# Rewriting the opening of an attention, dense and routed feed-forward kernel: all four units loaded at once, eight PSUM banks, and weight splitting moved behind it

## The reference, cut to what matters

```python
# attention: B=4, H=8, S=768, D=48, a linear recurrence with decay w per head and channel
for t in range(S):
    kt, vt, rt = (k[:, :, t], v[:, :, t], r[:, :, t])
    cur = np.einsum('bhd,bhe->bhde', u[None] * kt, vt)
    y[:, :, t] = np.einsum('bhd,bhde->bhe', rt, state + cur)
    state = w[None, :, :, None] * state + np.einsum('bhd,bhe->bhde', kt, vt)
# dense part: 3072 tokens, 384 -> 2048 -> 384
h = np.maximum(x @ w_in, 0.0);  x = h * h @ w_out
# routed part: 8 experts, 384 tokens each by capacity, 384 -> 1024 -> 384
h = np.maximum(x[mask] @ w1[e], 0.0);  out[mask] = h @ w2[e]
```

## Time and profile before

| | us |
|---|---|
| median of 3 runs | 879.27 (878.26 to 884.58) |
| the profiled execution | 880.52 |
| its span | 878.7 |
| PE busy | 841.0 (96%) |
| DVE busy | 514.7 (59%) |
| ACT busy | 261.2 (30%) |
| POOL busy | 229.2 (26%) |
| mean granted clock of TensorE | 0.978 of full |

### The profile page before, as it was taken

How to read it: one execution, slowest core, us unless ns; L and a number is a source line. 1 busy time by engine, 2 the same in 40 slices (tenths; PEclk the granted TensorE clock), 3 DMA queues, 4 the chain that set the end, 5 groups by cost and what they waited for, 6 DMA issues and landing times.

```text
span 878.7 us, 15962 instructions
## 1 busy us (share of the span) xinstructions
PE 841.0 (96%) x6289; PEld 730.1 (83%) x6289; DVE 514.7 (59%) x1143; ACT 261.2 (30%) x479; POOL 229.2 (26%) x197
## 2 busy tenths in 40 slices
PE   7789999999999999999999999987999999999895
PEld 7678888888888888888888888877988989889795
DVE  7657645666566557666666444546667667666220
ACT  1223323333333333333433344310121222222221
POOL 5545332322243314222323400001031131131211
PEclk9779999999999999999999999988999999999998
DMA  6553212665655565555654455524664674674940
GB/s 209 180 168 89 72 58 87 196 200 190 202 191 194 194 217 185 201 196 195 200 198 150 146 187 186 188 78 150 232 228 155 225 259 153 226 252 138 361 142 28
DMA packets 64300, 156.08 MB, mean 178 GB/s; under 512 B 8289, under 2 KB 13793, under 8 KB 63841
## 3 DMA queue, kind: packets, MB, share of 16 engines
q1 hardware_dynamic: 57696, 140.90, 47.2%
q0 software_dynamic: 3072, 9.44, 3.3%
q10 hardware_dynamic: 3456, 4.72, 1.5%
HBM read 103.65 MB, written 51.38 MB: 176 GB/s over the span
## 4 chain that ended last, share of the span: by engine, by line
PE 87%; DMA 5%; DVE 3%; issue 2%; SPq 1%; ACT 1%; POOL 1%; POOLq 0%; ACTq 0%; DVEq 0%
PE ACC L1251 23%; PE U L1238 23%; PE U L1379 10%; PE ACC L1392 9%; PE P L1201 5%; PE P L1185 3%; PE P L1311 3%; DMA stage<-in_ew 3%; PE P L1198 2%; PE P L1226 1%; PE P L1209 1%; DMA stage<-in_w_in 1%; PE P L1215 1%; DMA rk<-x_rows,rowidx 1%; PE P L1136 1%
## 5 line engine op out<-in xcount | busy, mean ns | idle before, releaser
L859 DVE TENSOR_TENSOR hr<-hr 128x512 f32<-128x512 f32 x96 | 69.6, 725 | 123.6 <-ACT hr L675 123.0
L675 ACT ACTIVATE hr<-U 128x512 f32<-128x512 f32 x96 | 57.3, 597 | 240.9 <-PE U L1238 240.9
L1251 PE MATMUL ACC<-HH,WH 128*128 128x512 f32 x282 | 117.3, 416 | 0.0
L1238 PE MATMUL U<-XH,WH 128*128 128x512 f32 x288 | 114.7, 398 | 1.2 <-DVE XL L838 1.2
L1238 PE MATMUL U<-XL,WH 128*128 128x512 f32 x288 | 114.3, 397 | 0.0
L1238 PE MATMUL U<-XH,WL 128*128 128x512 f32 x288 | 114.1, 396 | 0.0
L1251 PE MATMUL ACC<-HH,WL 128*128 128x512 f32 x282 | 111.5, 395 | 0.0
L1251 PE MATMUL ACC<-HL,WH 128*128 128x512 f32 x282 | 111.0, 394 | 0.0
L583 POOL TENSOR_TENSOR tok<-tok,sdiag 128x384 f32<-128x384 f32 x24 | 30.5, 1272 | 246.2 <-DVE sdiag L865 246.2
L874 DVE TENSOR_TENSOR HL<-hr,HH 128x512 fp32r<-128x512 f32 x96 | 75.8, 789 | 21.8 <-ACT HH L659 21.6
L628 POOL DMA_INDIRECT rk<-x_rows,rowidx x24 | 24.9, 1039 | 230.5 <-DVE rowidx L1030 225.6
(11 more groups left out here) (178 smaller groups left out, 1580.3 us busy)
## 6 DMA issues: line engine op xcount, KB each, us to landing
stage<-in_ew SPq DMA_DIRECT2D x80, 256.0 KB, 3.0
split_high<-stage SPq DMA_DIRECT2D x80, 256.0 KB, 2.0
split_low<-stage SPq DMA_DIRECT2D x80, 256.0 KB, 2.1
WH<-split_high SPq DMA_DIRECT2D x40, 512.0 KB, 5.8
WL<-split_low SPq DMA_DIRECT2D x40, 512.0 KB, 6.7
tok<-in_tok SPq DMA_DIRECT2D x24, 576.0 KB, 5.8
rk<-in_rk SPq DMA_DIRECT2D x24, 448.0 KB, 5.0
stage<-in_ew SPq DMA_DIRECT2D x8, 512.0 KB, 10.3
```

What stands on the lines that cost most here:

```text
L675: nc.scalar.activation(hr[:, s % 2, :], U[s % 2][:, :], ACT.Relu).then_inc(relu_done, 1)
L859: tt(hr[:, s % 2, :], hr[:, s % 2, :], hr[:, s % 2, :], ALU.mult).then_inc(sq_done, 1)
L1238: ins = mm(U[s % 2][:, :], w_up((WH, WL)[a], k, s), (XH, XL)[b][:, q, k, :], start=(n == 0), stop=(n == 3 * KT - 1))
L1251: ins = mm(ACC[j][:, :], w_down((WH, WL)[a], s, j), (HH, HL)[b][:, s % HRING, :], start=(s == 0 and a == b), stop=(s == NF1 - 1 and a == 1))
```

## The change

The opening becomes code of its own, and `blocks` starts at body(1).

- **Loads.** Right after w, SP issues unit 0, u, the two masks and units 1 to 3. Units 2 and 3 have buffers borrowed for it (`hr`, the second stage buffer), and one weight chunk follows. Constants that only later stages use come last.
- **Tables.** The reciprocal over 112 x 512 goes; the second table is the first one read backwards, times a number per row. The copy goes too, since the scan writes the table directly. `Wt` is copied out of PSUM by ACT.
- **Banks.** Scores of even units go to P[0:2], of odd ones to U; Y has P[2], the state ACC[0], transposes ACC[1], warm-ups ACC[2]. AT has a second buffer.
- **State.** In the opening the state is zero: the product with S, `Sd` and the addition of the state go. ACT copies the update into S.
- **Weights.** The host lays them out by tile (`dw`); eight chunks of 1536 columns, up and down in turn. Chunk 0 is split in the opening, chunks 1 to 7 in block 1 at steps 0, 1, 3, 5, 6, 8 and 10. PE waits for chunk n ahead of its first use, at step 2n. In block 1, `load_unit(4)` and `(5)` are issued in the opening.

```diff
-WARM_UP = (104, 40, 24)
+WARM_UP = (72, 6, 16)
         def chunk_at(s, att, moe, post):
-            if att and not moe and s % 4 == 1:
-                return s // 4
-            if att and moe and not post and s % 4 == 0 and BATCH + s // 4 < W1CHUNKS:
-                return BATCH + s // 4
+            if moe and not post:
+                return {0: 1, 1: 2, 3: 3, 5: 4, 6: 5, 8: 6, 10: 7}.get(s)
             return None
@@ SP
-            load_unit(0, 0, 0)
-            load_unit(1, 1, 1)
-            load_weights(0)
-            load_weights(1)
-            load_weights(2)
-            for b in range(2, BATCH):
-                sp.wait_ge(y_mm, b - 1)
-                load_unit(b, b % 2, b)
-                load_weights(b + 1)
+            load_unit(1, 1, 1)
+            for b in range(2, BATCH):
+                sp.dma_start(opening_rk(b)[0:KP]..., rk_in[b, :, :]).then_inc(ld_late[b % 2], 16)
+                sp.dma_start(tok[:, b, :, :]..., tok_in[b, :, :]).then_inc(ld_tok[b], 16)
+            load_weights(0)
...
+            sp.wait_ge(y_mm, BATCH)
+            load_weights(1)
+            load_weights(2)
+            load_weights(3)
+            load_weights(4)
+            next_unit(1, 2)
+            load_weights(5)
+            next_unit(1, 3)
+            load_weights(6)
+            load_weights(7)
@@ DVE, tables
-            nc.vector.tensor_copy(pw[:, 0, :, :], pwx[:, :, 0:CHUNK]).then_inc(tab, 1)
-            nc.vector.reciprocal(pw[:, 1, :, :], pwx[:, :, 1:CHUNK + 1]).then_inc(tab, 1)
+            tt(wend[:, :], ends, wT[:, :], ALU.mult).then_inc(tab, 1)
+            nc.vector.reciprocal(winv[:, :], wend[:, :]).then_inc(tab, 1)
+            tt(w128[:, :], w64[:, :], wend[:, :], ALU.mult).then_inc(tab, 1)
+            tt(winv[:, :], winv[:, :], w64[:, :], ALU.mult).then_inc(tab, 1)
+            tt(pw[:, 1, :, :], pw[:, 0, :, ::-1], winv[:, :].unsqueeze(2).broadcast_to([KP, PAIRS, CHUNK]),
                ALU.mult).then_inc(tab, 1)
@@ DVE, opening (order of its queue)
+            opening_scale(0)
+            tt(etab, ...)
+            opening_scale(1)
+            opening_mask(0)
+            diagonal(0, 0)
+            opening_mask(1)
...
@@ PE, opening
+            for b in range(BATCH):
+                opening_y(b)
+                opening_state(b)
+                warm_up(WARM_UP[1], ACC[2])
+                if b + 2 < BATCH:
+                    opening_at_scores(b + 2)
+                if b == 0:
+                    pe.wait_ge(wt_done, 2)
+                opening_transpose(b)
+            warm_up(WARM_UP[2], ACC[2])
```

More of the change, by code:

```diff
@@ L216, in bass_attention_moe_routed_moe @@
         ld_const = sem("ld_const")
+        ld_urow = sem("ld_urow")
+        ld_masks = sem("ld_masks")
+        ld_late = [sem(f"ld_late{i}") for i in range(2)]
+        wt_done = sem("wt_done")
+        ones_set = sem("ones_set")
         ld_stage = [sem(f"ld_stage{i}") for i in range(2)]
@@ L320, in tasks_of @@
         def tasks_of(att, moe, post):
[L322 to L330, removed]
             if not att:
@@ L574, in unit @@
                 nc.gpsimd.tensor_tensor(r_t, r_t, urow[:, :], ALU.mult).then_inc(rku_done, 1)
+                if not state:
+                    pool.wait_ge(wt_done, 2)
                 after(pool, st_mm, u)
@@ L791, in _ @@
[L791 to L797, removed]
+            tt(wend[:, :], ends, wT[:, :], ALU.mult).then_inc(tab, 1)
+            dve.wait_ge(tab, 13)
@@ L839, in task, with diagonal @@
                        XH[cols].bitcast(f32), ALU.subtract).then_inc(xlo_done, 1)
+            def diagonal(c, b):
+                u = BATCH * c + b
+                dve.wait_ge(rku_done, u + 1)
+                after(dve, sv_done, u)
+                nc.vector.tensor_reduce(sdiag[:, :], tok[:, b, 0, :].rearrange(
+                    "p (h d) -> p h d", d=HDIM), AX.X, ALU.add).then_inc(sdiag_done, 1)
             def scale(c, b):
@@ L860, in body @@
                     if diagonal_at(s, att, moe) is not None:
[L861 to L866, removed]
+                        diagonal(c, diagonal_at(s, att, moe))
                     for n, kind, b in tasks_at(s, att, moe, post):
@@ L1136, in warm_up @@
                     mm(bank[:, 0:128], onesb[:, :], onesb[:, :], start=True, stop=True)
[L1138 to L1147, removed]
+            pe.wait_ge(ones_set, 1)
+            warm_up(WARM_UP[0], ACC[2])
             def evacuated(c, kind, b):
@@ L1163, in evacuated, with scores @@
                     pe.wait_ge(lg_done, u - 2 * BATCH + 1)
+            def scores(u, r_t, k_t, banks):
+                pe.wait_ge(scaled, u + 1)
+                for p in range(PAIRS):
+                    for par in range(2):
+                        lo = HP * par
+                        ins = mm(banks[par][:, p * 128:(p + 1) * 128], k_t[lo:lo + HDIM, p, :],
+                                 r_t[lo:lo + HDIM, p, :], start=True, stop=True)
+                        if p == PAIRS - 1:
+                            ins.then_inc(at_mm, 1)
@@ new lines, in state_update, with transpose_y @@
+            def state_update(u, bank, v_t):
+                pe.wait_ge(kw_done, u + 1)
+                for h in range(HEADS):
+                    lo, cols = HP * (h % 2), slice(h * HDIM, (h + 1) * HDIM)
+                    ins = mm(bank[lo:lo + HDIM, cols], KW[:, h, 0:HDIM], v_t[:, cols],
+                             start=True, stop=True)
+                ins.then_inc(st_mm, 1)
+            def transpose_y(u, bank):
+                pe.wait_ge(yadd_done, u + 1)
+                for k in range(KT):
+                    ins = nc.tensor.transpose(bank[:, k * 128:(k + 1) * 128],
+                                              ysum[:, k * 128:(k + 1) * 128], ident[:, :])
+                ins.then_inc(tr_mm, 1)
@@ new lines, in opening_at_scores, with opening_y @@
+            def opening_at_scores(b):
+                if b >= 2:
+                    pe.wait_ge(at_done, 2 * (b - 2) + 2)
+                scores(b, opening_rk(b)[:, 0], opening_rk(b)[:, 1], opening_scores(b))
+            def opening_y(b):
+                pe.wait_ge(at_done, 2 * b + 2)
+                pe.wait_ge(ld_tok[b], 16)
+                after(pe, yadd_done, b)
+                for h in range(HEADS):
+                    cols = slice(h * HDIM, (h + 1) * HDIM)
+                    ins = mm(P[2][:, cols], opening_at(b)[:, h, :], tok[:, b, 2, cols], start=True, stop=True)
+                ins.then_inc(y_mm, 1)
@@ new lines, in opening_state, with opening_transpose @@
+            def opening_state(b):
+                after(pe, st_done, b)
+                state_update(b, ACC[0], tok[:, b, 2, :])
+            def opening_transpose(b):
+                after(pe, xlo_done, b)
+                transpose_y(b, ACC[1])
+            opening_at_scores(0)
+            pe.wait_ge(tab, TAB_STEPS)
+            pe.wait_ge(ld_masks, 16 * 2)
+            for p in range(PAIRS):
+                ins = nc.tensor.transpose(ACC[1][:, p * KP:(p + 1) * KP], etab[:, p, :], ident[0:KP, 0:KP])
@@ L1178, in task @@
                 if kind == "AT1":
[L1180 to L1185, removed]
-                                     r_t[lo:lo + HDIM, p, :], start=True, stop=True)
-                            if p == PAIRS - 1:
-                                ins.then_inc(at_mm, 1)
+                    scores(u, r_t, k_t, (P[(n - 1) % 3], P[n % 3]))
                 if kind == "Y":
-                    if isinstance(u, int) and u < BATCH:
-                        warm_up(WARM_UP[2])
                     pe.wait_ge(at_done, 2 * u + 2)
                     pe.wait_ge(ld_tok[b], 16 * (c + 1))
-                    after(pe, st_done, u - BATCH + 1)
+                    pe.wait_ge(st_done, u - BATCH + 1)
                     for p in range(PAIRS):
```

190 lines of the change are left out of this document (120 added, 70 removed).

## The result

| | before | after |
|---|---|---|
| median of 4 runs | 880.45 us | 869.93 us |
| ratio of after to before | | 0.9888, 95% interval 0.9861 to 0.9914 |
| profiled execution | 880.52 us | 872.64 us |
| its span | 878.7 us | 870.8 us |
| mean granted clock of TensorE | 0.978 | 0.965 |

The change makes the kernel 1.1% faster. The forecast was 856 with a range of 850 to 868: the sign was right, the size was not, and the time lies above the range.

What follows compares the result with a forecast made beforehand. Block 1 was taken as bound by PE, the opening before it by waits on a round trip per unit. 880.5 - 21.8 (opening) - 2.6 (clock), block 1 at nothing, gave 856 us, range 850 to 868.

Steps and rivals of the forecast that it cites:

- The clock: First dense matmuls and the scores behind them: full clock instead of 1.2 GHz, gain 2.6 us, bounds 0 and 3.3.
- The clock stays at 1.2 GHz: Opening, alternative in the nearly serial rival: start at 40, no clock gain, 865 us; chance 0.2 with all of 861 to 870.
- more than 6 us for unit after unit: Opening: the prediction named units taking more than 6 us each as a sign that it is wrong.
- are hidden, but for the first: Opening loads: all four units there by about 16 us at 353 GB/s, before unit 3's scale at about 21.
- the sum: Opening, VectorE and GpSimd in turns: 8.6 + 15.5 + 3.7 + 0.7 + 1.7 + 0.8 = 31.0 us to GpSimd's last product.
- The pace with turns: Opening: VectorE operations with both inputs in SBUF and GpSimd's exclude each other; first dense matmul at 33.6, gain 21.8 us.
- running free: Opening rival: VectorE and GpSimd overlap, VectorE's 4.2 us per unit sets the pace; start at 30, 852 us, chance 0.13.
- The split of chunk 0: Opening: one split of 1536 columns, 2.56 us beside GpSimd, counted as some 1.7 us in the turns.
- Tables: Start of the opening: scan ends at 5.93, plus 0.76 and 0.69 for the reversed product, done at 7.4 us.
- Block 1 at nothing: Block 1: seven weight splits instead of three, hidden on VectorE and ScalarE, with no PE wait; priced at nothing.
- Behind the dense part: After block 1: the prediction expected the time there to be as long as now.
- cold start: First nine dense matmuls: 4.21 us at half clock against 2.10 later; full clock was to give 2.1 back.

## Why the prediction was wrong, step by step

- **The clock** is the step that failed: "Now PE has fewer and shorter gaps ... I take full clock. Gain 2.6." It was priced only at the first dense matmuls and the scores behind them. There it gave 1.4 (4.21 to 2.81) and 0.9 (the scores of unit 4: 1.09 in the chain above, 2.01 in that of before, below), in all 2.3. That this is near 2.6 is luck, as the clock was at 0.50 for the 30 us ahead and not full at the start. What the forecast left out is that the change also takes warm-ups out of the opening: 32 at the start, the 40 behind them and 18 of 24 for each unit. Two gaps of 2.0 and 2.8 us were left, the clock fell at 10.7 us, and six warm-ups per unit did not bring it back. Filling the gaps gave 7.7 us (43.56 to 35.88). "The clock stays at 1.2 GHz" was half of a rival, priced as a lost gain of 2.6 and a slower hand-over. Its true price was PE's own time: 7.69 us a unit at half clock, where the forecast had GpSimd set the pace with 3.87 + 1.22 = 5.1. The sign that the prediction itself had named, more than 6 us for unit after unit, came true.

```profile
59.62 2.01 PE P L1185 x16
```

- **Loads "are hidden, but for the first"** failed as well, and made the second gap. The r and k of units 0 to 3 landed 3.8, 7.2, 9.9 and 14.2 us after their issue, each behind the others in the queue. The 7.2 are those of unit 1: VectorE waits 2.3 us for them, PE 2.8, and the masks and sdiag of unit 0 stand behind that scale. With the gaps filled VectorE still waits 3.1 us there and GpSimd 2.8 for sdiag, where the sum had 0.8 in all. I used 353 GB/s; the windows above have 262 to 290 with the DMA share at 1.0, and the last tok, issued at 6.9, took 14.6 us and landed at about 21.5 instead of 16. Units 2 and 3 were in time in the changed kernel; with the gaps filled VectorE waited 0.2 us for unit 2.
- **The pace with turns** was right in kind where the clock held, and a little dear. With the gaps filled a unit takes GpSimd 4.65 us (its product of v and sdiag starts at 15.40, 20.05 and 24.71), between the 4.2 of running free and the 5.1 of the sum. The scale of unit 2 and the product beside it:

```profile
16.76 1.51 DVE L1073 TENSOR_TENSOR hr<-hr,pw 112x1024 f32<-112x1024 f32 x1 [0.24 <-DMA hr<-in_rk]
17.27 1.86 POOL L577 TENSOR_TENSOR tok<-tok,urow 128x384 f32<-128x384 f32 x1
```

GpSimd's product ahead of these ended at 17.19, the scale 1.08 later, at 18.27, and the next product 0.86 after that, at 19.13. The Trainium skill (SBUF — State Buffer; Who interferes with whom) says that an instruction of VectorE with two inputs in SBUF contends with one of GpSimd that reads SBUF, and that one of the two blocks fully. These rows agree with that.

- **The split of chunk 0** was priced at 1.7 us of turns, not at its place. In VectorE's queue it stands ahead of a ysum, and PE waits 2.4 us for that ysum with the gaps filled. The load, 17.5 us from issue to landing, held ScalarE up by only 0.5, and the wait was as long where the split came later. Behind the wait the clock fell again. How much of 35.9 - 33.6 = 2.3 us is due to this and how much to unit 1's load was not measured.
- **Tables** done at 7.3, as forecast (7.4); the reversed read costs 0.69, the low end.
- **Block 1 at nothing**: no wait of PE there. But the dense part got 1.5 us longer by a cause that I had not thought of, the addresses.
- **Behind the dense part** the profiled run after lost another 4.8 us: from the first logits to the end of the span 303.0 against 298.2 before. 2.2 of it is the clock at the last long wait of the experts, where nine matmuls took 3.25 and 2.43 instead of 1.85 and 1.59. The second profile of the kernel before has 3.25 and 2.73 there, so this fall is not the change's doing. The versions of the changed kernel on chips of this speed have 299.5 to 303.0 from the logits on; of the kernel before there is only the one profile with 298.2, and on the slower chip both kinds have 311 to 312. Whether the change has a part in the other 2.6 stays open.

Together: -11.9 (start) - 2.3 (cold start) + 1.5 (addresses) + 4.8 (behind) = -7.9, and the profiled executions differ by 880.5 - 872.6 = 7.9. Against the forecast of 856 the profiled run is 16.6 too long: 10.0 at the start (43.56 instead of 33.6), 0.3 at the cold start, 1.5 and 4.8.

## What to carry to other kernels

When a change shortens or thins PE's work ahead of a stage that is not yet bound by PE, work out that stage twice, with PE's durations at either clock, and look for every stretch in which PE will stand still. Warm-ups belong where PE waits: here six per unit started the dense blocks later (43.56) than none (41.26) or 24 (38.72). A transfer that stood behind others in its queue landed late, at 14.2 us for the fourth unit against 3.8 for the first, and an engine that waits for one in program order holds up what stands behind.

## What the runs showed of the hardware that was not expected

- The small matmuls of the attention, back to back for 30 us and called busy, left the clock at 0.50. It was 1.00 again in the window from 45.0 us, behind the start of the dense groups, and in the run with 24 warm-ups per unit within the first burst.
- The clock fell behind waits of quite different length: a wait of 1.9 us with a busy stretch behind it did not drop it in one run, while one of 0.9 us for the scale of unit 2 was followed by a fall in another. In a run with the same code up to there that wait was 0.6 us, and the clock held.
- Moving all later tiles by 32 bytes changed the dense part by 0.3% in one direction (523.8 against 522.3 us) and the experts by 0.4% in the other (33.18 against 33.32 us each).
- The same kernel took 880 us on some chips and 890.6 on another, with the difference in the routed part (35.3 against 33.3 us per expert) and none in the opening (55.33 against 55.41).
